# Attention and two MLPs on one core: another order of the launch, one load of values split in another way, and one conversion of weight sums moved

## The reference

```python
k_sum = k.reshape(B, H, nb, 32, D).max(axis=3)        # largest key of each block of 32
v_sum = v.reshape(B, H, nb, 32, D).mean(axis=3)       # mean value of each block
scores_l = scale * q @ k.T, kept where |i - j| < 16, else -1e9
scores_s = scale * q @ k_sum.T + log(32)
a = softmax(concat(scores_l, scores_s)); x = a @ concat(v, v_sum)
x = x.transpose(0, 2, 1, 3).reshape(B * S, H * D)
xn = x / rms(x) * rms_g
g, val = xn @ w_gate, xn @ w_val                      # 512 -> 1536
x2 = (g * sigmoid(g) * val) @ w_out                   # 1536 -> 512
h = x2 @ w_in; out = (h - tanh(h)) @ w_out2           # 512 -> 2048 -> 512
```

## Time and profile before

| | us |
|---|---|
| median of 3 runs | 629.43 |
| lowest and highest | 628.95 and 630.87 |
| the profiled execution | 630.87 |
| its span, first to last instruction | 629.1 |
| what lies around the span | 1.8 |
| PE busy (share of the span) | 612.3 (97%) |
| DVE, ACT, POOL busy | 428.1, 323.9, 170.3 |
| granted TensorE clock, mean | 0.994 |

### The profile page before, as it was taken

One profiled execution on the slowest core, in us unless ns is written; L12 is line 12 of the kernel. 1 busy time (PEld: TensorE's weight loads), 2 busy tenths in 40 slices (PEclk: granted clock), 3 DMA queues, 4 the chain that ended last, 5 costly groups with the idle time before them and its releaser, 6 DMA issues.

```text
span 629.1 us, 10688 instructions
## 1 busy us (share of the span) xinstructions
PE 612.3 (97%) x3972; PEld 568.6 (90%) x3972; DVE 428.1 (68%) x697; ACT 323.9 (51%) x622; POOL 170.3 (27%) x223
## 2 busy tenths in 40 slices
PE   7789999999999999999999999999999999999997
PEld 7468889999999998889898899999999989898986
DVE  3688667667753449877777689999543597666643
ACT  5485554445433327555555467776332375555542
POOL 4474612021210203322220545662200222222200
PEclk9799999999999999999999999999999999999999
DMA  8998913312311121222222162222313023222102
GB/s 242 191 230 149 213 50 94 79 28 80 93 51 51 52 68 50 68 68 73 64 71 66 49 198 67 68 68 71 97 54 115 0 72 97 67 68 68 33 2 100
DMA packets 96210, 53.90 MB, mean 86 GB/s; under 512 B 33760, under 2 KB 90336, under 8 KB 95968
## 3 DMA queue, kind: packets, MB, share of 16 engines
q1 hardware_dynamic: 95728, 52.44, 31.8%
q10 hardware_dynamic: 432, 0.79, 0.3%
HBM read 50.07 MB, written 3.15 MB: 85 GB/s over the span
## 4 chain that ended last, share of the span: by engine, by line
PE 86%; DVE 4%; ACT 3%; POOL 3%; issue 2%; DMA 2%; SPq 0%; DVEq 0%; POOLq 0%; ACTq 0%
PE bank L929 11%; PE bank L933 11%; PE bank L931 11%; PE bank L872 10%; PE bank L874 10%; PE bank L873 10%; PE bank L1038 7%; PE bank L1037 7%; PE bank L1036 7%; PE bank L856 1%; DMA k_rows<-in_k_dram 1%; POOL sm L608 1%; PE bank L836 1%; PE bank L807 1%; PE bank L817 1%
## 5 line engine op out<-in xcount | busy, mean ns | idle before, releaser
L1696 DVE TENSOR_TENSOR h_lo<-pd,h_hi 128x384 fp32r<-128x384 f32 x112 | 71.0, 635 | 27.8 <-ACT h_hi L1423 13.9
L1038 PE MATMUL bank<-y_hi,h_lo 128*128 128x512 f32 x192 | 75.5, 393 | 0.0
L1037 PE MATMUL bank<-y_lo,h_hi 128*128 128x512 f32 x192 | 75.4, 393 | 0.0
L1036 PE MATMUL bank<-y_hi,h_hi 128*128 128x512 f32 x192 | 75.3, 392 | 0.0
L696 POOL TENSOR_TENSOR ws_raw<-x_raw 128x256 f32<-128x256 f32 x16 | 11.8, 740 | 209.2 <-PE bank L933 127.6
L872 PE MATMUL bank<-h_hi,z_hi 128*128 128x384 f32 x192 | 64.9, 338 | 0.0
L874 PE MATMUL bank<-h_hi,z_lo 128*128 128x384 f32 x192 | 64.5, 336 | 0.0
L873 PE MATMUL bank<-h_lo,z_hi 128*128 128x384 f32 x192 | 64.5, 336 | 0.0
L1290 ACT CAST h_hi<-pd 128x384 fp32r<-128x384 f32 x48 | 24.7, 514 | 44.2 <-DVE pd L1726 32.3
L1407 ACT COPY part<-bank 128x384 f32<-128x384 f32 x48 | 22.9, 478 | 43.3 <-PE bank L933 42.2
L1038 PEld LDWEIGHTS bank<-y_hi,h_lo 128*128 128x128 f32 x192 | 36.0, 188 | 8.2
(11 more groups left out here) (207 smaller groups left out, 1719.1 us busy)
## 6 DMA issues: line engine op xcount, KB each, us to landing
x_raw<-in_moe_w_in_dram SPq DMA_DIRECT2D x32, 256.0 KB, 3.4
y_raw<-in_moe_w_out_dram SPq DMA_DIRECT2D x32, 256.0 KB, 2.7
x_raw<-in_moe_w_gate_dram SPq DMA_DIRECT2D x24, 256.0 KB, 3.6
y_raw<-in_moe_w_val_dram SPq DMA_DIRECT2D x24, 256.0 KB, 3.3
z_raw<-in_moe_w_out_dram SPq DMA_DIRECT2D x16, 384.0 KB, 3.6
k_rows<-in_k_dram SPq DMA_DIRECT2D x8, 384.0 KB, 5.3
qn<-in_q_dram SPq DMA_DIRECT2D x12, 256.0 KB, 7.7
vw_early<-in_v_dram SPq DMA_DIRECT2D x12, 192.0 KB, 5.3
```

The source lines that it names most:

```text
L1036: nc.tensor.matmul(AB[t][:], a_hi, w_hi, start=begins, stop=False, skip_group_check=True)
L1037: nc.tensor.matmul(AB[t][:], a_hi, w_lo, start=False, stop=False, skip_group_check=True)
L1038: last = nc.tensor.matmul(AB[t][:], a_lo, w_hi, start=False, stop=ends, skip_group_check=True)
L1696: nc.vector.tensor_tensor(dst, full, high.bitcast(f32), ALU.subtract).then_inc(done, 1)
```

## The change

1. PE, launch: the products that keep the clock up are 30 ahead of the first pair of K and 2 between pairs, where they were 7, 0, 5 and 3 ahead of the four pairs.
2. PE: `block_sums` stands ahead of `scores(1)`, not behind it; the queries of a tile are transposed one tile earlier (tile 2 ahead of the loop, T + 3 in it).
3. ACT: the first `means` goes between the two exponentials of tile 0, and the copies of the queries move one tile earlier.
4. DVE: `pair_values` comes ahead of the two `shift` of tile 0; the fourth pair of K is arranged after the first `block_maxima`.
5. SP: the first tiles of the gate and value weights, x and y 0 and 1, are issued earlier, the loads of values 3 to 5 alternate with those of the second K, and `blk` comes in two DMAs of 96 partitions x 2048 numbers (L523) in the place of four of 24 partitions x 2 x 2048.
6. ACT, `up_pair`: S1 and S2 of VAL of the next pair are converted right behind the four sums of GATE, ahead of `high_up` and of the saving after P6 on GATE; S3 and S4 move from behind the saving on VAL to ahead of it.

```diff
--- before.py
+++ after.py
@@ -49,7 +49,7 @@
     k_p = k.rearrange("b h (p r) d -> b p h (r d)", r=ROWS)
     v_p = v.rearrange("b h (p r) d -> b p h (r d)", r=ROWS)
     v_v = v.rearrange("b h s d -> b s h d")
-    v_b = v.rearrange("b (c h) (n t) d -> b c n h (t d)", h=2, t=BLOCK)
+    v_b = v.rearrange("b (c h) (n t) d -> b h c n (t d)", h=2, t=BLOCK)
     gate_v = moe_w_gate.rearrange("(c p) f -> p c f", p=P)
     val_v = moe_w_val.rearrange("(c p) f -> p c f", p=P)
     down_v = moe_w_out.rearrange("(j p) n -> p j n", p=P)
@@ -506,23 +506,21 @@
             load_q(2)
             load_values(1)
             load_q(3)
+            load_xy(0)
+            load_q(4)
+            load_values(2)
             sp.dma_start(g_bc[:, :], g_v).then_inc(g_in, 16)
-            load_values(2)
-            load_q(4)
-            load_xy(0)
-            load_values(3)
             load_q(5)
-            load_values(4)
+            load_xy(1)
             sp.wait_ge(k_arranged, PAIRS)
             for c in range(PAIRS):
-                if c == 2:
-                    load_values(5)
-                    load_xy(1)
+                if c < 3:
+                    load_values(3 + c)
                 sp.dma_start(k_rows[:, 2 * c:2 * c + 2, :], k_p[1][:, 2 * c:2 * c + 2, :]).then_inc(k_in[c], 16)
             load_q(TPB)
             sp.wait_ge(means_mm, 1)
-            for c in range(KC):
-                sp.dma_start(blk[c * NBLK:(c + 1) * NBLK, :, :], v_b[1, c]).then_inc(blk_in, 16)
+            for hf in range(2):
+                sp.dma_start(blk[:, hf, :], v_b[1, hf]).then_inc(blk_in, 16)
             for t in range(1, TPB):
                 load_q(TPB + t)
             for m in range(2):
@@ -664,7 +662,7 @@
                                             ALU.subtract).then_inc(x_lo_done, 1)
             inverse_rms(TPB - 2)
             inverse_rms(TPB - 1)
-            pool.wait_ge(blk_in, 16 * KC)
+            pool.wait_ge(blk_in, 32)
             add_blocks()
             pool.wait_ge(k1_copied, ROWS)
             move_windows(TPB)
@@ -1107,19 +1105,22 @@
                 units(1 if i == 1 else 2)
 
             pe.wait_ge(ident_done, 1)
+            keep_clock_up(30)
             for c in range(PAIRS):
-                keep_clock_up((7, 0, 5, 3)[c])
                 transpose_k(c)
+                if c < PAIRS - 1:
+                    keep_clock_up(2)
             transpose_q(0)
             transpose_q(1)
             scores_in_place()
+            block_sums()
             scores(1)
-            block_sums()
+            transpose_q(2)
             for T in range(TPB):
                 if 2 <= T + 1 < TPB:
                     scores(T + 1)
-                if T + 2 < TPB:
-                    transpose_q(T + 2)
+                if T + 3 < TPB:
+                    transpose_q(T + 3)
                 if T == TPB - 1:
                     gate(0, 0, 0)
                 transpose_probs(T, 0)
@@ -1360,13 +1361,12 @@
                     split_z(ZG + 1)
                 if i + 1 < J1 // 2:
                     split_up_sums(i + 1, GATE)
+                    split_up_sums(i + 1, VAL, slice(S1, S3))
                 high_up(i, "C11")
                 keep_up(i, "P6", GATE)
                 if i + 1 < J1 // 2:
-                    split_up_sums(i + 1, VAL, slice(S1, S3))
+                    split_up_sums(i + 1, VAL, slice(S3, 4))
                 keep_up(i, "P6", VAL)
-                if i + 1 < J1 // 2:
-                    split_up_sums(i + 1, VAL, slice(S3, 4))
                 keep_up(i, "P7", GATE)
                 keep_up(i, "P7", VAL)
                 tanh_up(i, "C22")
@@ -1471,12 +1471,13 @@
             copy_q(0)
             copy_q(1)
             exp(0, 0)
-            exp(0, 1)
             act.wait_ge(means_mm, 1)
             means(vw_early[:, 0], TX).then_inc(means_act, 1)
+            exp(0, 1)
             copy_q(2)
             copy_probs(0, 0)
             copy_probs(0, 1)
+            copy_q(3)
             for slot in (1, 2):
                 means(vw_early[:, slot], TX).then_inc(means_act, 1)
             for T in range(1, TPB):
@@ -1488,8 +1489,8 @@
                 exp(T, 1)
                 copy_probs(T, 0)
                 copy_probs(T, 1)
-                if T + 2 < TPB:
-                    copy_q(T + 2)
+                if T + 3 < TPB:
+                    copy_q(T + 3)
                 square(T - 1)
                 if T == 2:
                     split_x(0)
@@ -1952,14 +1953,16 @@
                 add_total(p, "C12", "P3", 3 * p + 2, part[:, 1, :], VB)
                 low_tile(p, "C21")
 
-            for c in range(PAIRS):
+            for c in range(3):
                 arrange_k(0, c)
             for c in range(PAIRS):
                 dve.wait_ge(k_copied, c + 1)
                 block_maxima(0, c)
+                if c == 0:
+                    arrange_k(0, 3)
+            pair_values()
             shift(0, 0)
             shift(0, 1)
-            pair_values()
             for T in range(1, TPB):
                 shift(T, 0)
                 if T == TPB - 1:
```

## The result

| | before | after |
|---|---|---|
| median of 4 runs, us | 629.44 | 636.54 |
| lowest and highest | 628.95, 630.87 | 635.62, 638.28 |
| profiled execution, us | 630.87 | 635.82 |
| its span | 629.1 | 634.1 |
| granted clock, mean | 0.994 | 1.000 |

By these medians the changed kernel takes 7.1 us more, by the two profiled spans 5.0. Of the changed kernel 26 executions are on record, from 635.04 to 641.32 us with a median of 637.3; the ratio of the times is taken over all of them and is 1.0125, with a 95% interval of 1.0094 to 1.0155: 7.9 us more. The forecast was 635.6.

A forecast was written before the change was run, and what follows sets the result against it. PE's matmuls were taken as the bound from 90 us on, a latency chain before that. Profiled 630.87 + 1.2 (launch) + 3.5 (first MLP of row 1), loads nothing, made 635.6 us; range 630.8 to 643.0, with 0.50 on 633.5 to 637.5.

The follow-up runs named there:

- b_undo: The changed kernel with the load of blk put back to four DMAs of 24 partitions: 635.28 us, ratio 1.0087 to the kernel before.

## What to carry to other kernels

When an instruction is moved ahead on an in-order engine, look at what it waits for and count the work that it now holds back behind that wait: that work, and not the wait, is the delay of whoever reads it. When a load gets slower, look past its reader, at the next loads in the same issuing queue. A launch that gets faster has to be followed to the next thing that comes by itself, here the weights near 70 us; otherwise the time is won and given back.

## What the runs showed that was not expected

- *The clock's phase differs from one execution to the next.* The same 60 passes took 9.54 us in one kernel and 8.43 in another, and the block sums of the old order 3.33, 3.35, 4.23, 4.81 and 5.32 us in five traces, by where the fall and the return to 2.4 GHz came. With the arrival of K's third pair, this moves `weigh_values` between 24.78 and 27.68 us in them. A profiled execution shows one draw of it, and the prediction was made against the latest but one.
- *A second fall at 83 us, which cost nothing.* Where PE waited 2.25 to 3.02 us for the queries behind the late `x_raw`, the clock read 0.50 for about 3 us afterwards, and products came every 0.32 us for 0.17. With a wait of 2.08 us (the kernel with the new order and eight products) it stayed at 1.00.
- *An engine moved the same rows at twice the rate in the new form.* Both forms are 192 packets of 8 KB, one row of one partition each; in the packets' own times one takes 0.31 us in the new form and 0.6 in the old one, as medians. So a third of the engines needs only 3 to 4 us more for `blk`, and what is lost is the room for others: 106 GB/s in all from 50 to 58 us, against 150 before and 191 in `b_undo`. Why an engine is slower in the old form, whether by its 24 partitions or by the loads beside it, was not tried.
- *What lies around the span* is 1.7 to 1.8 us in every run of every kernel without products in the gap, and 1.8 to 2.5 us in the four kernels with them. Part of their gain is lost there. The cause is open.
- *The wait of 0.78 us at 54.75 us* that no releaser explains stays open as well: it is in one trace only.
